# A 64-byte move of the intermediate activations in an attention, mixture-of-experts and feed-forward kernel

## The reference, cut to what matters

```python
    for e in range(E):
        for k in range(2):
            mask = top2[:, k] == e
            ...
            h = np.maximum(x[mask] @ w1[e], 0.0)
            out[mask] += top2_w[mask, k, None] * (h @ w2[e])
...
    h = x @ w_in
    g = h - np.tanh(h)
    return (g @ w_out).astype(np.float32)
```

## Time and profile before

| | |
|---|---|
| median of 3 runs | 2085.78 us (2084.58 to 2087.2) |
| the profiled execution: its time, its span | 2084.23 us, 2082.5 us |
| granted TensorE clock, mean over the span | 0.969 |
| PE busy, PEld busy | 1941.1 us (93%), 1750.1 us (84%) |
| DVE, ACT, POOL busy | 1074.2, 837.0, 562.2 us |
| matmuls | 13280 |

### The profile page before, as it was taken

How to read it: one execution, slowest core, us unless ns; L and a number is a source line. 1 busy time by engine, 2 the same in 40 slices (tenths; PEclk the granted TensorE clock), 3 DMA queues, 4 the chain that set the end, 5 groups by cost and what they waited for, 6 DMA issues and landing times.

```text
span 2082.5 us, 36878 instructions
## 1 busy us (share of the span) xinstructions
PE 1941.1 (93%) x13280; PEld 1750.1 (84%) x13281; DVE 1074.2 (52%) x2002; ACT 837.0 (40%) x1776; POOL 562.2 (27%) x527
## 2 busy tenths in 40 slices
PE   6887882899999999999999996999999999999999
PEld 5676772798989999999998986889999889999888
DVE  6888865313131313223131315766677766677765
ACT  4665663323232323223232324544444444444444
POOL 3255354122222211221221212222322222322222
PEclk9998897899999999999999998999999999999999
DMA  8354332413131312213131312001100001100000
GB/s 219 104 143 109 108 80 81 143 51 132 48 133 45 113 64 76 95 50 121 44 138 40 136 45 102 31 31 41 49 30 30 30 30 40 51 30 30 30 30 21
DMA packets 79077, 152.34 MB, mean 73 GB/s; under 512 B 12768, under 2 KB 37472, under 8 KB 76224
## 3 DMA queue, kind: packets, MB, share of 16 engines
q1 hardware_dynamic: 62720, 108.42, 16.6%
q0 software_dynamic: 16320, 43.45, 6.3%
HBM read 111.51 MB, written 40.33 MB: 73 GB/s over the span
## 4 chain that ended last, share of the span: by engine, by line
PE 86%; DVE 7%; issue 2%; DMA 2%; POOL 1%; ACT 1%; SPq 0%; DVEq 0%; POOLq 0%; ACTq 0%
PE banks L707 13%; PE banks L705 13%; PE banks L706 13%; PE banks L696 12%; PE banks L697 12%; PE banks L698 12%; PE banks L686 3%; PE banks L593 2%; PE banks L572 2%; PE banks L612 1%; PE banks L581 1%; POOL slot_row L469 1%; DVE idxf L1105 1%; DVE kp L1014 1%; DMA v_raw<-in_v 1%
## 5 line engine op out<-in xcount | busy, mean ns | idle before, releaser
L696 PE MATMUL banks<-x_hi,w_hi 128*128 128x256 f32 x2304 | 639.1, 277 | 5.3 <-DVE x_lo L1224 4.1
L698 PE MATMUL banks<-x_hi,w_lo 128*128 128x256 f32 x2304 | 638.5, 277 | 0.0
L697 PE MATMUL banks<-x_lo,w_hi 128*128 128x256 f32 x2304 | 638.5, 277 | 0.0
L705 PE MATMUL banks<-w_hi,h_hi 128*128 128x512 f32 x1184 | 467.2, 395 | 3.0 <-DVE h_lo L1248 3.0
L707 PE MATMUL banks<-w_hi,h_lo 128*128 128x512 f32 x1184 | 466.1, 394 | 0.0
L706 PE MATMUL banks<-w_lo,h_hi 128*128 128x512 f32 x1184 | 463.1, 391 | 0.0
L696 PEld LDWEIGHTS banks<-x_hi,w_hi 128*128 128x128 f32 x2304 | 434.9, 189 | 8.2 <-DVE x_lo L1224 4.9
L697 PEld LDWEIGHTS banks<-x_lo,w_hi 128*128 128x128 f32 x2304 | 434.8, 189 | 2.5
L698 PEld LDWEIGHTS banks<-x_hi,w_lo 128*128 128x128 f32 x2304 | 434.7, 189 | 0.0
L534 POOL TENSOR_SCALAR large<-u_sq 128x512 uint8<-128x512 f32 x144 | 222.4, 1545 | 585.2 <-ACT u_sq L963 317.6
L1231 DVE SCALAR_TENSOR_TENSOR h_lo<-banks,h_hi 128x512 fp32r<-128x512 f32 x144 | 99.6, 691 | 379.6 <-ACT h_hi L914 379.6
(11 more groups left out here) (141 smaller groups left out, 2270.0 us busy)
## 6 DMA issues: line engine op xcount, KB each, us to landing
w_raw<-in_moe_w SPq DMA_DIRECT2D x32, 1024.0 KB, 5.2
y<-y_rows SPq DMA_DIRECT2D x18, 1024.0 KB, 5.0
k_raw<-in_k SPq DMA_DIRECT2D x32, 288.0 KB
q_sb<-in_q SPq DMA_DIRECT2D x32, 288.0 KB, 7.0
v_raw<-in_v SPq DMA_DIRECT2D x8, 1152.0 KB
x_rows<-x_sb SPq DMA_DIRECT2D x32, 288.0 KB, 3.7
out_x<-y_sb SPq DMA_DIRECT2D x36, 256.0 KB, 2.1
w_raw<-in_moe_w_in SPq DMA_DIRECT2D x4, 1024.0 KB, 4.8
```

Of the source, the lines that this page charges most:

```text
L696: pe.matmul(part, hi, x_hi[:, c, :], start=(c == 0), stop=False)
L697: pe.matmul(part, hi, x_lo[:, c, :], start=False, stop=False)
L698: mm = pe.matmul(part, lo, x_hi[:, c, :], start=False, stop=(c == NC - 1))
L705: pe.matmul(p_y[m][:, :], hi, w_hi[par][:, o:o + DM], start=(j == 0), stop=False)
```

## The change

The tiles are placed in another order. Nothing else changes: each of the five engines runs the same instructions in the same order, with the same shapes, and only addresses in SBUF differ.

- `large` (512 bytes), `c_w0` (160) and `idx_g` (32) now lie behind the weights, 704 bytes together, in place of `c_w`, `idx_g`, `idx_s` and the spacer. `y2`, `x_hi` and `x_lo` keep their addresses.
- A spacer of 64 bytes now lies between `x_lo` and `h_hi`. `h_hi` and `h_lo` start 768 bytes behind the weights modulo 4096 in place of 704. `y_sb`, `u_sq` and `th` move up by 64 bytes with them.
- `large` has left its place between `th` and `g32`, so `g32` moves down by 448 bytes; `c_w1` and `idx_s` lie behind it.

```diff
         w_hi.append(sb("w_hi1", [128, WE], f32r))
         w_lo.append(sb("w_lo1", [128, WE], f32r))
-        c_w = [sb(f"c_w{i}", [128, TC]) for i in range(2)]
+        large = sb("large", [128, 2 * NB], mybir.dt.uint8)
+        c_w = [sb("c_w0", [128, TC])]
         idx_g = sb("idx_g", [128, SUB], i32)
-        idx_s = sb("idx_s", [128, SUB], i32)
-        sb("spacer", [128, 80])
         y2 = sb("y2", [128, SUB, 2 * DM])
         xg = y2[:, :, 0:DM]
         x_hi = sb("x_hi", [128, NC, NB], f32r)
         x_lo = sb("x_lo", [128, NC, NB], f32r)
+        sb("spacer", [128, 16])
         h_hi = sb("h_hi", [128, FT2, NB], f32r)
         h_lo = sb("h_lo", [128, FT2, NB], f32r)
         y_sb = sb("y_sb", [128, SUB, DM])
         u_sq = [sb(f"u_sq{i}", [128, 2 * NB]) for i in range(2)]
         th = sb("th", [128, 2 * NB])
-        large = sb("large", [128, 2 * NB], mybir.dt.uint8)
 
         rows_all = u_sq[0][:, 0:COLS + 2 * SUB].bitcast(i32)
         toks_all = th[:, 0:COLS + 2 * SUB].bitcast(i32)
         g32 = [sb(f"g32_{i}", [128, 2 * NB]) for i in range(2)]
+        c_w.append(sb("c_w1", [128, TC]))
+        idx_s = sb("idx_s", [128, SUB], i32)
```

## The result

| | median | runs |
|---|---|---|
| before | 2086.27 us (2084.58 to 2087.21) | 6 |
| changed | 2107.39 us (2104.06 to 2108.70) | 6 |

The changed kernel takes 1.010 times the time of before (95% interval 1.009 to 1.0111): 21.1 us more, slower, and outside the range of 2065 to 2100 that was given. The experiments ran in four groups; each is compared with runs of the kernel before on the same chip, where that took 2085 us for two groups and 2134 us for the other two (the additional 48 us lie ahead of the expert stage: its first product starts at 373 to 379 us in the traces of the first two groups, at 422 to 426 us in those of the others). So experiments are told by their ratio, and by rates read from their traces.

What follows compares the result with a forecast made beforehand. PE's matmul rate in `up` and `down` was taken as the bound. All terms were 0 us, added to 2084.23 us profiled; the median to compare was 2085.8 us, with a range of 2065 to 2100 us for 8 in 10.

Steps and rivals of the forecast that it cites:

- The stationary operand of `down`: In `down`, moving `h` from 704 to 768 bytes costs 0 ns per matmul; bounds 55 us gain, 24 us loss.
- The first: In `down`, durations don't scatter over addresses modulo 4096, so only the distance within 512 bytes can matter.
- The second: In `down` and half blocks, durations 388, 392, 394 follow the place in a round of three, not the operands.
- the nearest row: Half blocks' first product, with `x` as stationary operand at the same 704 bytes, taken to say no change.
- The third: `up` pays 6.7 ns above its columns, `down` 15.5, so the excess looks like the stream's, not the load's.
- `up`: 0 us, since its addresses stay: In `up`, weights and `x` keep their addresses, so the change costs 0 us.
- if `up` moves although its addresses stay: Sign that the prediction is wrong, beside `down`'s start-to-start distance moving by more than 1.2 ns.
- Better distance: Rival: `down` gets faster at 256 than at 192 bytes within 512, 2 to 4 ns per matmul, 2075 us; chance 0.29.
- prices of 38, 46 and 55 us: Possible `down` gains: the transposes' rate (38), a skill-page estimate (46), its whole excess of 15.5 ns per matmul (55).
- Worse distance: Rival: `down` slows as both reads run in step; 2.7 ns gives 2095 us, 6.7 gives 2110; 0.21 including a new bound.
- Another engine becomes the bound: Rival: slower DVE reads show in the first dense block, a few us at most; chance 1 in 50.
- The tiles of DVE, ACT and POOL and the DMAs: Tile work hidden behind PE, 0 us; DMAs 0 us, 0.3 either way, from one output transfer on the path.

Runs made afterwards that it cites:

- h960: Changed kernel with 256 bytes between `x_lo` and `h_hi` in place of 64, so `h` lies 960 bytes behind the weights; ratio to before 0.9993.
- kick64: Changed kernel with one more matmul of 64 columns ahead of each `up` of a full block; ratio to before 1.0000.
- mid_kick: Changed kernel with an added matmul of 64 columns in the middle of each `up` of the expert and dense blocks; ratio to before 1.0070.
- order_alone: Changed kernel without its 64-byte spacer: tiles in the new order, `h` again 704 bytes behind the weights; ratio to before 0.9995.
- kick64_before: Kernel before with one more matmul of 64 columns ahead of each `up` of a full block; ratio to before 1.0041.
- all_plus64: Changed kernel with 64 bytes ahead of the first weight tile, moving weights, `x` and `h` together; ratio to before 1.0119.
- x768_h768: Changed kernel with its 64-byte spacer ahead of `y2`, so `x` and `h` both lie 768 bytes behind the weights; ratio to before 1.0175.
- x768_h768_kick64: Changed kernel with `x` and `h` both at 768 bytes, plus a matmul of 64 columns ahead of each `up` of a full block; ratio to before 1.0197.
- split_last: Changed kernel with the last matmul of each full block's second product split into two of 256 columns; ratio to before 0.9977.
- up_order: Changed kernel with the second and third matmul exchanged in all triples of `up`; ratio to before 1.0091.
- swap_first: Changed kernel with the second and third matmul exchanged only in the first triple of each `up`; ratio to before 1.0106.

## Why the prediction was wrong

**What bounds the kernel** was right: PE's rate in `up` and `down`, and nothing else. A small change of either is paid in full, several thousand times.

**The stationary operand of `down`: 0 ns.** Wrong: it is 2.2 ns per matmul, 8 us, to the faster side, next to the 7 us that the rate of `up` gave as a bound for a gain. Of the three points behind it:

- The first, that nothing repeats at 4096 bytes and only the distance within 512 can matter, held. h960 narrows it to 256, for the pair 704 and 960.
- The second, that the three durations go with the place in a round and not with the operands, was a true reading and a wrong conclusion. The order within the round says nothing of the addresses. The mean of the three medians does: it is 391.3 ns in the earlier trace rows and in the earlier trace rows, where `h` and `x` lay at the same distance, and 390.0 at 768. I called the half blocks the nearest row. They were no second distance, and could not tell.
- The third, that an excess that grows with the streamed columns is no matter of the load, fell: at 736 and 832 the same columns cost 4.3 ns more.

**`up`: 0 us, since its addresses stay.** This is the step that failed, at 29 us. Nothing that `up` reads was moved, and still it went from 113.4 to 117.8 ns. It has two steady rates at the same addresses, and what runs just before it decides which one: kick64 (same addresses, 21 us less), mid_kick (both rates in one product) and the three blocks behind unsplit half blocks show it. So the move of `h` reached `up` through what runs before it, most likely the changed pace of `down`. That last link is inferred: no row shows the hand-over itself. The prediction listed this very sign at its end, "if `up` moves although its addresses stay", without a rival for it.

**The rivals.** "Better distance" was right about `down`, with 2.2 ns where I would have said 2 to 4. No distance tried brought `down` below 226.7 ns, so of the prices of 38, 46 and 55 us, which want 10.8 ns and more, nothing past the first 8 us was there. "Worse distance" had the right sign, and its prices of 2095 and 2110 us lie around the 2107 measured, but that is luck: it put the loss on `down`, which became faster, and had `up` stay. Its reason, that 256 bytes as an even part of 512 bring the two reads into step, came out the other way for `down`: 768 is the best distance tried, and 736 and 832 to both sides of it are the bad ones, at 4.3 and 4.4 ns more than 704. "Another engine becomes the bound" did not happen. The tiles of DVE, ACT and POOL and the DMAs were costed at nothing. order_alone confirms it to 0.15% for `large`, `g32`, `c_w` and the indices; for `y_sb`, `u_sq` and `th`, h960 does, where they lie 256 bytes further on and the ratio is 0.9993.

**The pages.** "TensorE: Matmul & The Clock Gate" in the Trainium skill, "Step-by-step: what each phase is for", says that the load takes nothing from the running matmul. Here the distance of the two reads changes `down` between 226.8 and 233.4 ns, so the measurement decides against it for float32r operands.

**What stays open.** Whether the distance counts modulo 256 beyond the one pair tried, and why, and why just 0 is best for a stationary piece and bad for the streamed `x`. What tells the two rates of `up` apart inside the chip: 113.4 is half of 226.8 and 117.8 is half of no rate seen. Why `up` runs at 113.4 with the split at 768 and 896 and not at 832, what let kick64_before slip in two blocks, and what picks the rate in the first expert block, where either comes. So a step of another length is a try, not a rule. Of x only two distances were tried.

## What to carry to other kernels

Where PE runs without gaps, read start-to-start distances of its matmuls before and after every change, for each product apart, also for those the change doesn't touch: the stream can have more than one steady rate at the same addresses, and what runs before can decide. If a product slows down though none of its operands moved, try a step of another length at the hand-over, such as one matmul split in two, before judging the change. And two rows that agree are no evidence that a quantity doesn't matter when both have the same value of it; ask which row has another.

## What the runs showed of the hardware

- With float32r operands, the distance between the stationary piece that is loaded and the weights that stream changes the rate: per 512 columns 226.7 to 227.1 ns at 768 bytes, 229.0 at 704 and 960, 232.4 at 896, and 233.3 to 233.4 at 736 and 832. Moving weights, `x` and `h` together by 64 bytes (all_plus64) leaves both rates; moving `h`, with the tiles behind it, from 704 to 960 (h960) does too.
- 256 columns of `x` past loaded weights take 120.0 ns at 768, with or without a 64-column matmul ahead (x768_h768, x768_h768_kick64). At 704 they take 113.4 or 117.8 ns, each steady over 96 or 192 matmuls. With `h` at 768, one matmul of 64 columns (kick64, mid_kick) or a split one (split_last) takes the stream from the slow to the fast rate; exchanging the operands of neighbouring matmuls (up_order, swap_first) does not.
